# Routed experts on 32-token tiles in plain fp32, four column groups of TensorE, weights in a ring of five experts

## What is computed

```python
B, H, S, D = 2, 8, 768, 64           # block-sparse attention
scores_l = scale * q @ k.T           # kept where |i - j| < 16
scores_s = scale * q @ k_max.T + log(32)   # k_max: maximum over blocks of 32 keys
a = softmax(concat(masked scores_l, scores_s));  x = a @ concat(v, v_mean)   # 1536 tokens x 512

do_compute = x @ w_skip > 0          # routed experts: E = 8, 512 -> 1024 -> 512
e_idx = argmax(x[do_compute] @ w_gate)
y = gate * (relu(x @ w1[e]) @ w2[e]) # for the tokens of expert e
x = x + y                            # tokens that are skipped keep x

h = x @ w_in;  g = h * cos(h);  out = g @ w_out    # 512 -> 2048 -> 512
```

## Time and profile before

| | us |
|---|---|
| median of 3 runs | 580.46 (580.17 to 583.71) |
| the profiled execution: span, first to last instruction | 580.3 |
| attention, to the transposes of the logits | 0 to 107.3 |
| routing and dispatch, to the first expert product | 107.3 to 141.5 |
| experts, to their last product | 141.5 to 280.5 |
| to the first `out_slot` | 280.5 to 315.7 |
| the last two layers | 315.7 to 580.3 |

### The profile page before, as it was taken

One profiled execution on the slowest core, in us unless ns is written; L12 is line 12 of the kernel. 1 busy time (PEld: TensorE's weight loads), 2 busy tenths in 40 slices (PEclk: granted clock), 3 DMA queues, 4 the chain that ended last, 5 costly groups with the idle time before them and its releaser, 6 DMA issues.

```text
span 580.3 us, 9279 instructions
## 1 busy us (share of the span) xinstructions
PE 512.9 (88%) x2829; PEld 417.8 (72%) x2830; DVE 400.4 (69%) x626; ACT 288.3 (50%) x591; POOL 115.0 (20%) x122
## 2 busy tenths in 40 slices
PE   4788899553989999889956999999999999999996
PEld 4667666252777777777945888888888888888885
DVE  7777864451694848999947767667776676766664
ACT  2666767601653537677634444445444444444442
POOL 3343434085141303333540000000000000000000
PEclk9989999766999999999968999999999999999999
DMA  9989999834772827989872000000300000100001
GB/s 208 247 198 232 242 230 306 309 118 153 278 276 108 325 81 295 354 325 357 334 239 113 19 19 20 12 7 18 127 0 0 0 0 0 73 1 1 0 1 72
DMA packets 58012, 82.66 MB, mean 142 GB/s; under 512 B 17324, under 2 KB 35500, under 8 KB 57984
## 3 DMA queue, kind: packets, MB, share of 16 engines
q1 hardware_dynamic: 56064, 78.28, 42.0%
q0 software_dynamic: 1920, 4.03, 2.5%
HBM read 65.42 MB, written 17.56 MB: 143 GB/s over the span
## 4 chain that ended last, share of the span: by engine, by line
PE 63%; DMA 11%; DVE 8%; issue 7%; SPq 5%; ACT 3%; POOL 2%; DVEq 1%; POOLq 0%; ACTq 0%
PE bank L1182 19%; PE bank L1184 18%; PE bank L1183 18%; DMA raw<-weights 5%; DMA q_blockdiag<-q_T 5%; DVE w_lo L901 3%; PE bank L1104 2%; PE bank L1059 2%; POOL rows_sorted L518 2%; PE bank L1079 1%; DVE hT_lo L930 1%; DMA v_window<-v_sum 1%; ACT prob L551 1%; SPq L311 1%; SPq L292 1%
## 5 line engine op out<-in xcount | busy, mean ns | idle before, releaser
L901 DVE TENSOR_TENSOR w_lo<-raw,w_hi 128x1024 fp32r<-128x1024 f32 x62 | 101.5, 1670 | 18.6 <-ACT w_hi L632 15.8
L1182 PE MATMUL bank<-w_hi,gT_hi 128*128 128x512 f32 x192 | 75.9, 395 | 5.7 <-DVE gT_lo L1007 5.7
L632 ACT ACTIVATE w_hi<-raw 128x1024 fp32r<-128x1024 f32 x70 | 70.0, 1051 | 17.3 <-DMA raw<-weights 13.7
L1182 PE MATMUL bank<-x2T,w_hi 128*128 (+1 forms) x192 | 76.6, 399 | 1.6 <-DVE x2T L970 1.6
L1184 PE MATMUL bank<-w_hi,gT_lo 128*128 128x512 f32 x192 | 75.7, 394 | 0.0
L1183 PE MATMUL bank<-w_lo,gT_hi 128*128 128x512 f32 x192 | 75.7, 394 | 0.0
L1184 PE MATMUL bank<-x2T,w_lo 128*128 (+1 forms) x192 | 75.3, 392 | 0.0
L1183 PE MATMUL bank<-x2T,w_hi 128*128 (+1 forms) x192 | 75.3, 392 | 0.0
L712 ACT ACTIVATE turns<-reduced,half_pi 128x512 f32<-128x512 f32 x48 | 34.8, 724 | 74.0 <-DVE reduced L998 74.0
L705 ACT ACTIVATE turns<-bank,quarter 128x512 f32<-128x512 f32 x48 | 33.1, 689 | 69.2 <-PE bank L1184 69.2
L511 POOL TENSOR_TENSOR w_lo<-raw,w_hi 128x1024 fp32r<-128x1024 f32 x18 | 45.8, 2545 | 104.4 <-ACT w_hi L632 81.1
(11 more groups left out here) (145 smaller groups left out, 965.5 us busy)
## 6 DMA issues: line engine op xcount, KB each, us to landing
raw<-weights SPq DMA_DIRECT2D x80, 512.0 KB, 6.4
rows_sorted<-zeros SPq DMA_DIRECT2D x7, 768.0 KB, 5.7
k_padded<-k_T SPq DMA_DIRECT2D x8, 384.0 KB, 5.7
q_blockdiag<-q_T SPq DMA_DIRECT2D x16, 192.0 KB, 4.9
v_tok<-v_pairs SPq DMA_DIRECT2D x8, 384.0 KB, 6.0
v_window<-v_pairs SPq DMA_DIRECT2D x8, 384.0 KB, 4.4
x_plain<-x_tok SPq DMA_DIRECT2D x1, 3072.0 KB, 9.8
xs_in<-rows_sorted SPq DMA_DIRECT2D x12, 256.0 KB, 7.2
```

Source lines behind the costliest of these rows:

```text
L632: sc.activation(hi, raw[:, c, :], ACT.Copy).then_inc(hi_done, 1)
L901: v.tensor_tensor(lo, raw[:, c, :], hi.bitcast(F32), ALU.subtract).then_inc(lo_done, 1)
L1182: te.matmul(out_ap, a[0], b[0], start=start, stop=False)
```

## The change

- **Experts in 32-token tiles, fp32 as it is.** No hi and lo for expert weights. The first layer multiplies a stationary 128x32 tile of x with 256 columns of w1, four times beside each other: each of four products writes its own 32 output partitions (a column group of the array) and has its own quarter of the hidden columns. The second layer does the same with 128 columns. It runs one tile late, behind the first layer of the next.
- **A ring of five whole experts** in on-chip memory, raw. Two are loaded during attention, two chunks a pair; the next three after it; three experts, `w_in` and `w_out` as slots come free. `w_in` and `w_out` are split after the last expert, the later chunks inside the first group of the last layers.
- **Dispatch by gathering.** x is stored plainly, a pair at a time, during attention. After the slots are known an inverse permutation (token of each slot) is made with one-hot products on TensorE, and GpSimd gathers fourteen blocks of 128 rows from it.
- **Attention's buffers shrink** to make room: v_tok has one buffer, q goes through one contiguous buffer `q_raw` and is placed by GpSimd.
- The loops of attention and of the last layers are written out.

Cut to its core, the constants first:

```diff
+
+MT = 32
+CG = P // MT
+FG = FF // CG
+JC = FG // P
+THR = NTOK // MT
+MAXT = THR + E - 1
+NBLK = -(-MAXT * MT // P)
+ZROW = NBLK * P
+SLOTS = 5
 F2 = 2048
```

On SyncE:

```diff
+            def load_q(i):
+                ge(sp, q_placed, i)
+                sp.dma_start(qraw[:, :], qT[i, :, :]).then_inc(q_loaded, 16)
+
+            def load_vtok(i):
+                ge(sp, vs_ready, i)
+                sp.dma_start(vtok[:, :, :], v2[i, :, :].rearrange("(t p) d -> p t d", p=P)).then_inc(vtok_loaded, 16)
+
...
+            def store_x(i):
+
+                sp.wait_ge(xt_copied, GPP * i + GPP)
+                dst = xd.rearrange("(b t p) (c f) -> p b t c f", b=B, t=TPB, c=PPB)
+                sp.dma_start(dst[:, i // PPB, :, i % PPB, :], xstage[i % 2][:, :, :]).then_inc(x_stored[i % 2], 16)
+
+            def load_chunk(src, s, c):
+                sp.dma_start(wslot[s][:, c, :], weights[NCH * src + c, :, :]).then_inc(w_loaded[s][c // 4], 16)
+
...
+            for i in range(PAIRS):
                 sp.wait_ge(keys_ready, i + 1)
-                if not first:
+                if i + 2 < PAIRS:
+                    load_k(i + 2)
+                    load_q(i + 2)
+                if i > 0:
                     sp.wait_ge(xps_ready, GPP * i)
-                load_windows(i + 1, 1 - par)
-                place_vsum(i + 1, 1 - par)
-                sp.wait_ge(scores_ready, GPP * i + GPP)
-                load_chunk(0, c)
+                if i + 1 < PAIRS:
+                    load_windows(i + 1)
+                    place_vsum(i + 1)
+                if i + 2 < PAIRS:
+                    load_vtok(i + 2)
+                for n in range(BESIDE * i, BESIDE * (i + 1)):
+                    load_chunk(n // NCH, n // NCH, n % NCH)
+                if i > 0:
+                    store_zeros(i - 1)
+                if i > 1:
+                    store_x(i - 2)
+            store_x(PAIRS - 2)
+            store_x(PAIRS - 1)
...
+            sp.wait_ge(x_kept, STEPS - GPP)
+            sp.wait_ge(last_kept, GPP)
+            sp.wait_ge(zero_stored, 16 * PAIRS)
+            for e in range(BESIDE, SLOTS):
+                for c in range(NCH):
+                    load_chunk(e, e, c)
+            sp.wait_ge(gate_ready, 1)
+            sp.wait_ge(idx_ready, 1)
...
+            for done, src, s in ((1, 5, 0), (2, 6, 1), (3, 7, 2), (4, E, 3), (6, E + 1, 0)):
+                sp.wait_ge(expert_done, done)
+                for c in range(NCH):
+                    load_chunk(src, s, c)
```

On GpSimd:

```diff
+            def place_q(i):
+
+                pool.wait_ge(q_loaded, 16 * i + 16)
+                ge(pool, scores_ready, GPP * i - GPP)
+                q3 = qraw[:, :].rearrange("p (t q) -> p t q", q=QT)
+                g.tensor_scalar(qbd[i % 2][:, :, 0:QT], q3, head_mask[:, 0:1], None, ALU.mult)
+                g.tensor_scalar(qbd[i % 2][:, :, QT:2 * QT], q3, head_mask[:, 1:2], None, ALU.mult).then_inc(q_placed, 1)
...
+            for s in range(2):
+                primed(pool, x_stored[s], 16 * (PAIRS // 2))
+            pool.wait_ge(idx_ready, 1)
+            for k in range(NBLK + 2):
+                if k < NBLK:
+                    pool.indirect_dma_start(xg[:, k, :], None, xd,
+                                            bass.IndirectOffsetOnAxis(ap=idx[:, k:k + 1].bitcast(U32), axis=0))\
+                        .then_inc(gathered[k % 4], 16)
+                if k >= 2:
+                    pool.wait_ge(gathered[(k - 2) % 4], 16 * ((k - 2) // 4 + 1))
+                    pool.sem_inc(blocks_ready, 1)
+
...
+            primed(pool, y_stored, 16 * ntiles + 32)
+            pool.wait_ge(zero_stored, 16 * PAIRS)
...
+            for t in range(2 * TPG):
+                gather_y(t)
+            for c in SPLIT_POOL:
+                raw, hi, lo = split_parts(c)
+                pool.wait_ge(hi_done, HI_ORDER.index(c) + 1)
+                g.tensor_tensor(lo, raw, hi.bitcast(F32), ALU.subtract).then_inc(lo_pool, 1)
```

On ScalarE:

```diff
+            def copy_xT(n):
+
+                primed(act, t1_ready, n + 1)
+                primed(act, h_ready, n)
+                src = xb_ps[:, :].rearrange("p (c q r) -> p c q r", c=KC, q=CG)
+                sc.activation(xTt[:, :, :], src[:, :, bass.ds(n % CG, 1), :].rearrange("p c q r -> p c (q r)"), ACT.Copy)\
+                    .then_inc(xt_ready, 1)
+
+            def store_y(n):
+
+
+                primed(act, y_copied, n)
+                primed(act, y_stored, 16 * n + 16)
+                dst = rows[bass.ds((n - 1) * MT, MT), :].rearrange("r (g f) -> g r f", g=CG)
+                act.dma_start(dst, y_out[:, bass.ds((n - 1) % 2, 1), :].rearrange("p o f -> p (o f)")).then_inc(y_stored, 16)
+
+            def tile(n, stored):
+
+                primed(act, h_ready, n + 1)
+                primed(act, t2_ready, n)
+                sc.activation(hid[:, :], h_ps[:, 0:FG], ACT.Relu).then_inc(relu_done, 1)
+                copy_xT(n + 1)
+                if stored:
...
+            def high_part(c):
+
+                raw, hi, _ = split_parts(c)
+                sc.activation(hi, raw, ACT.Copy).then_inc(hi_done, 1)
+
+            act.wait_ge(expert_done, 5)
+            act.wait_ge(w_loaded[3][0], 128)
+            for c in range(4):
+                high_part(c)
+            act.wait_ge(expert_done, 8)
+            act.wait_ge(w_loaded[0][0], 192)
+            for c in (8, 9):
+                high_part(c)
```

On VectorE:

```diff
+            for s in range(2):
+                primed(dve, x_stored[s], 16 * (PAIRS // 2))
...
+            then(v.tensor_scalar(blk[:, :], rank[:, :], 1.0 / P, -0.5 + 0.5 / P, ALU.mult, ALU.add))
+            then(v.tensor_scalar(blk[:, :], blk[:, :], MAGIC, -MAGIC, ALU.add, ALU.add))
+            then(v.scalar_tensor_tensor(out=low[:, :], in0=blk[:, :], scalar=-float(P), in1=rank[:, :],
+                                        op0=ALU.mult, op1=ALU.add))
+            BLK = [P, NT, NBLK]
+            then(v.tensor_tensor(inblk[:, :, :], spread(blk[:, :], BLK), repeat(count[:, 0:NBLK], BLK), ALU.is_equal))
+            v.tensor_tensor(slot1h[:, :, :], spread(low[:, :], [P, NT, P]), repeat(count[:, :], [P, NT, P]),
+                            ALU.is_equal).then_inc(perm_ready, 1)
+            v.tensor_scalar(blkval[:, :, 0:NBLK], inblk[:, :, :], pcol[:, :], None, ALU.mult).then_inc(perm_ready, 1)
+            v.tensor_tensor(blkval[:, :, NBLK:2 * NBLK], inblk[:, :, :], spread(tnext[:, :], BLK), ALU.mult)\
+                .then_inc(perm_ready, 1)
             v.tensor_copy(slot[:, :], rank[:, :]).then_inc(slot_ready, 1)
+            dve.wait_ge(idx_summed, 1)
+            then(v.tensor_copy(idxf[:, :], idx_ps[:, 0:NBLK]))
+            then(v.scalar_tensor_tensor(out=idxf[:, :], in0=idx_ps[:, NBLK:2 * NBLK], scalar=float(P), in1=idxf[:, :],
+                                        op0=ALU.mult, op1=ALU.add))
+            v.tensor_scalar(idx[:, :], idxf[:, :], -float(P), 0.0, ALU.add, ALU.max).then_inc(idx_ready, 1)
...
+            def copy_block(n):
+
+                dve.wait_ge(blocks_ready, n // CG + 1)
+                primed(dve, t1_ready, n)
+                v.tensor_copy(xblk[:, :], xg[:, bass.ds(n // CG, 1), :].rearrange("p o f -> p (o f)"))\
+                    .then_inc(block_copied, 1)
+
+            def copy_y(n):
+
+
+                primed(dve, y_ready, n)
+                primed(dve, y_stored, 16 * n)
+                v.tensor_copy(y_out[:, bass.ds((n - 1) % 2, 1), :].rearrange("p o f -> p (o f)"), y_ps[:, 0:P]).then_inc(y_copied, 1)
+
+            def tile(n, stored):
+
+                copy_block(n + 1)
+                if stored:
+                    copy_y(n)
+                primed(dve, t2_ready, n + 1)
+                v.tensor_copy(hT[:, :, :], ht_ps[:, 0:JC * P].rearrange("p (j q) -> p j q", j=JC)).then_inc(ht_ready, 1)
```

On TensorE:

```diff
+            pe.wait_ge(perm_ready, 3)
+            for t in range(NT):
+                last = te.matmul(idx_ps[:, 0:2 * NBLK], slot1h[:, t, :], blkval[:, t, :], start=(t == 0), stop=(t == NT - 1))
+            last.then_inc(idx_summed, 1)
...
+            def transpose_block(n):
+
+                primed(pe, block_copied, n + 1)
+                for c in range(KC):
+                    last = te.transpose(xb_ps[:, P * c:P * (c + 1)], xblk[:, P * c:P * (c + 1)], ident[:, :])
+                last.then_inc(t1_ready, 1)
+
+            def first_product(n, e):
+
+                primed(pe, xt_ready, n + 1)
+                primed(pe, relu_done, n)
+                w = wslot[SLOT_OF[e]]
+                for c in range(KC):
+                    for g in range(CG):
+                        last = te.matmul(h_ps[MT * g:MT * (g + 1), 0:FG], xTt[:, c, :], w[:, c, FG * g:FG * (g + 1)],
+                                         start=(c == 0), stop=(c == KC - 1))
+                last.then_inc(h_ready, 1)
+
+            def second_product(n, e):
+
+
+                primed(pe, ht_ready, n)
+                primed(pe, y_copied, n - 1)
+                w = wslot[SLOT_OF[e]]
+                for k in range(CG * JC):
```

(41 more changed lines are left out.)

811 lines of the change are left out of this document (305 added, 506 removed).

## The result

The changed kernel takes 600.09 us (median of 4 runs, 597.67 to 604.31) beside 580.32 of the kernel before: a ratio of 1.031, 95% interval 1.023 to 1.039. The forecast was 551, range 528 to 588. The profiled execution of after has a span of 599.7 us.

The account below looks back on a forecast made before the run. TensorE was taken to bound the last layers (264.6 us, unmoved) and experts, a DMA-fed chain attention. From 580.3: attention +18, dispatch -3.3, experts -40.6, wait before last layers -5.6, last layers +2 gave 550.8, forecast 551 us, range 528 to 588.

Parts of the forecast that it names:

- Attention, the loss: Attention: one v_tok buffer makes rounds longer and GpSimd's q passes delay the start; +18 us, bounds +8 to +26.
- The start: Start of attention: GpSimd places q 0 before the masks and identity that the first sums need; 1.5 us.
- The rounds: Attention: windows, v_tok's landing, sums and two steps make 14.3 us a round; four rounds cost 3.1 us more each.
- The fifth round: Attention's round that also has the logits: 5.0 us more than before.
- GpSimd's two further passes stand within TensorE's wait: Attention: GpSimd's two extra passes a pair stand between two `normalise` but within TensorE's wait; no cost put on them.
- The queue sets a floor near this: Attention: DMA traffic, including expert weights and x, sets a floor of 13.5 to 14 us a round.
- Experts, the gain: Experts' stage: 18 tiles of 5.3 us, 98.4 us against 139.0; -40.6 us, bounds -53 to -22.
- Last layers: Last layers: GpSimd's ten low-part splits may delay VectorE's low parts; +2 us, bounds 0 to +8.
- Dispatch and the wait before the last layers: Dispatch to first expert product -3.3 us (-8 to +3); last expert product to first `out_slot` -5.6 us (-8 to -2).
- Two groups at a time: Rival, experts: only two column groups overlap, a tile takes 8.7 us, the whole 612 us; chance 0.12.
- four that gain less: Rival, experts: four column groups with products slowed by a quarter, 6.3 us a tile, +18, 569 us; chance 0.13.
- Attention no longer than before: Rival, attention: short wait for v_tok and a queue draining sooner, +1 instead of +18, 534 us; chance 0.13.

Follow-up runs that it names:

- e1: The changed kernel with two v_tok buffers, each load issued two pairs ahead: 576.2 us, ratio 0.986 to the kernel before.
- e6: e1 with both masked copies of q made by VectorE instead of GpSimd: 572.3 us, ratio 0.980 to the kernel before.
- e11: The changed kernel, one v_tok buffer kept, with no expert's weights loaded beside attention: 607.3 us, ratio 1.043 to the kernel before.
- e7: e6 plus the edits of e2 and e5 and a third x_stage buffer for the last pair: 555.7 us, ratio 0.955 to the kernel before.
- e13: The changed kernel without the stores of y and their waits, the experts' part of the output missing: 585.2 us, ratio 1.003 to the kernel before.
- e2: The changed kernel with GpSimd's ten low halves of the last layers' weights made by VectorE: 589.9 us, ratio 1.008 to the kernel before.
- e5: The changed kernel with four y_out buffers and two stores of y in flight from ScalarE: 589.7 us, ratio 1.011 to the kernel before.

## Why the prediction was wrong

The outline of each part was right, but three terms were mis-sized, attention by 25 us, the experts by 22 and the last layers by 6, all on the slow side. Inside the first two stand waits that the sum had at nothing: GpSimd's passes over q, the tail of attention, the landing of the store before, and TensorE's "issue" stalls.

**"Attention, the loss", +18: it was +42.9.** The order of the round was right, and its transfer too (5.2 to 6.5 us for 5.5). *The start*, put at 1.5, cost 11.3: I gave GpSimd's passes no price, though the step named them as ahead of the masks and the identity; they take 4.4 us for each pair, and the wait for v_tok of pair 1 comes on top. e1 took 4.3 of it back, e6 9.5 more. *The rounds*, put at 14.3, took 15.8 in the mean: 18.5 over before instead of 12.4. The difference is the clock, at 0.50 to 0.68 in the sums and the next step, which stood in the bounds as +1.7 a round: in the round shown the sums took 2.77 instead of 1.4 and the step behind them 3.8 instead of 2.5. I took the value without it, though a wait of 5 us for TensorE in every round was my own argument. *The fifth round* cost 8.4 instead of 5, and the *tail* 4.6 instead of nothing, where x_stage's two buffers wait for a store that SyncE issues behind weights; e11, without the weights, has the tail of before. The fifth round's excess and the tail were not in the sum. "GpSimd's two further passes stand within TensorE's wait" was right for after but for its start, and e1 and e6 show the passes in the chain once that wait is gone. "The queue sets a floor near this" was wrong: e11 has the same rounds with 8 MB fewer in the queue, and e6 and e7, with the same bytes as after, have shorter ones (10.7 to 14.6).

**"Experts, the gain", -40.6: it was -18.9.** The tile was priced too high (5.3, measured 4.70; the lower bound said 4.6): 11 us better than forecast, which by luck hid as much of the loss. But "ScalarE (relu, a copy, one DMA issue) ... hidden" counted the issue of the store and not its wait for the landing of the one before: 16.4 us by e13. `relu_done` is where TensorE waited, as the step said it would if ScalarE were late. The other part of the miss is what the sum had nowhere, the "issue" stalls and the slow products behind them: the stage of e13 is 103.4, 5 over the forecast, though its tiles are 11 under. That the stalls are code loading stays open. Weights never stopped the stage, as forecast.

**"Last layers", +2 (0 to +8): it was +7.6.** It lies inside the bound, at its end, but by another instruction: I looked at the split pieces, and the delay was in the `tensor_scalar` beside them, which costs five times its price in the chain. e2 gives all of it back.

**Dispatch and the wait before the last layers** were right to 2.2 and 1.1 us: counts read in 5.63 us for 5.9, `keep_warm` 8.86 for 9.0, `slot_one_hot` 1.76 for 1.6.

*The rivals.* "Two groups at a time" and "four that gain less" are refuted: 32 records of 256 columns, 0.22 us each one after another by my count, take 1.93 us, 3.6 times less. The Trainium skill (TensorE: Matmul & The Clock Gate, Part 3: Packing small matmuls) has 2.38 for three groups; this trace is closer to the full count. "Attention no longer than before" was the opposite of what came. No rival was a loss in attention beyond its bound together with waits on y; the chance of 0.15 for slower lay almost wholly on the column groups, the part of the change with the most to say and, as it came out, the safest.

## What to carry to other kernels

When a change gives a buffer up, write out the loop from the transfer through that buffer back to its own issue, with the slow clock in it, and then ask which work was hidden under the old wait: it is the next round's price. A store that is waited for before the next is issued costs its landing under load and not its size: have as many in flight as a landing has work steps, and look for the landings of small transfers that share the queues with big ones. Bandwidth that a stage has left is not free while small transfers of its chain queue behind what is put there.

## What I had not expected of the hardware

- Four column groups of plain fp32 run abreast almost without loss: 64 records of 128 columns in 1.93 to 1.98 us.
- VectorE's `tensor_scalar` of 128x512 goes from 0.42 us to between 2.15 and 2.37 beside a GpSimd `tensor_tensor`; the 1.7 to 1.9 us that it loses are more than a split takes on VectorE itself (1.22).
- A 64 KB store in 128 rows of 512 bytes lands after 1.0 to 2.7 us on ScalarE's queue with no weight loads about, and after 6.1 to 13.8 with them (after and e5); issued by GpSimd it comes round in 4.1 and 8.
- TensorE stood still for 1.8 to 4.8 us at three places of e13, two of them in the middle of a product, with transfers of the instruction queue about; it looks like code being fetched, which no run here tested.
